# Token mix of a fused attention and channel-mix kernel: U times the tokens in plain fp32 on 32-column tiles, summed by VectorE, and one product with V's high and low half on the partitions

## What is computed

```python
def _moe2_ref(x, U, V, w_ch1, w_ch2):          # x is (4, 576, 512), U (576, 32), V (32, 576)
    xt = x.transpose(0, 2, 1)
    h = xt @ U @ V                             # per batch: tokens reduced to 32 rows, and spread again
    u = x + h.transpose(0, 2, 1)
    ch = np.maximum(u @ w_ch1, 0.0) @ w_ch2
    return (u + ch).astype(np.float32)
```

## Time and profile before

| | |
|---|---|
| median of 3 runs | 800.24 us (797.22 to 801.04) |
| profiled execution | 798.4 us, its span 796.6 us |
| granted TensorE clock, mean | 0.994 of full speed |
| busy, TensorE / weight loads | 759.2 us (95%) / 666.6 us (84%) |
| busy, VectorE / ScalarE / GpSimd | 335.2 / 299.9 / 153.1 us |
| chain that ended last, TensorE's share | 87% |

### The profile page before, as it was taken

One profiled execution on the slowest core, in us unless ns is written; L12 is line 12 of the kernel. 1 busy time (PEld: TensorE's weight loads), 2 busy tenths in 40 slices (PEclk: granted clock), 3 DMA queues, 4 the chain that ended last, 5 costly groups with the idle time before them and its releaser, 6 DMA issues.

```text
span 796.6 us, 13313 instructions
## 1 busy us (share of the span) xinstructions
PE 759.2 (95%) x5040; PEld 666.6 (84%) x5040; DVE 335.2 (42%) x706; ACT 299.9 (38%) x787; POOL 153.1 (19%) x168
## 2 busy tenths in 40 slices
PE   4689899999999999899999999999999999999998
PEld 2567788888888888778899999899899889899997
DVE  6758776767576836765411211121131122113111
ACT  4647676666777655533433110110110111111110
POOL 5777220302011214300565100000000000000000
PEclk9979999999999999999999999999999999999999
DMA  7863342323233101000243100010010001001001
GB/s 141 198 159 61 66 78 47 62 53 70 43 60 62 51 1 53 1 27 1 82 132 105 38 2 1 1 39 0 0 39 0 0 0 39 0 0 41 1 0 40
DMA packets 121748, 35.77 MB, mean 45 GB/s; under 512 B 109536, under 2 KB 115680, under 8 KB 121696
## 3 DMA queue, kind: packets, MB, share of 16 engines
q1 hardware_dynamic: 112000, 34.02, 17.6%
q10 hardware_dynamic: 9696, 1.05, 0.9%
HBM read 30.33 MB, written 4.72 MB: 44 GB/s over the span
## 4 chain that ended last, share of the span: by engine, by line
PE 87%; DVE 6%; issue 2%; ACT 2%; SPq 1%; DMA 0%; ACTq 0%; DVEq 0%
PE bank L1193 27%; PE bank L1195 26%; PE bank L1194 26%; PE bank L1245 2%; PE bank L1234 2%; PE bank L1214 2%; SPq L471 1%; DVE sq L1051 1%; PE bank L1274 1%; DVE sq_l L1055 1%; DVE xf L1041 1%; PE bank L1333 1%; DVE probs L994 1%; PE bank L1347 1%; PE bank L1334 1%
## 5 line engine op out<-in xcount | busy, mean ns | idle before, releaser
L1163 DVE SCALAR_TENSOR_TENSOR h_l<-bank,h_h 128x384 fp32r<-128x384 f32 x96 | 53.5, 558 | 308.9 <-ACT h_h L933 308.9
L933 ACT ACTIVATE h_h<-bank 128x384 fp32r<-128x384 f32 x96 | 47.2, 492 | 333.5 <-PE bank L1195 333.4
L1193 PE MATMUL bank<-ut_h,w_h 128*128 128x384 f32 x384 | 130.5, 340 | 0.0
L1195 PE MATMUL bank<-ut_h,w_l 128*128 128x384 f32 x384 | 129.4, 337 | 0.0
L1194 PE MATMUL bank<-ut_l,w_h 128*128 128x384 f32 x384 | 129.0, 336 | 0.0
L1195 PE MATMUL bank<-w_h,h_l 128*128 128x512 f32 x288 | 113.8, 395 | 0.0
L1194 PE MATMUL bank<-w_l,h_h 128*128 128x512 f32 x288 | 113.6, 395 | 0.0
L1193 PE MATMUL bank<-w_h,h_h 128*128 128x512 f32 x288 | 112.0, 389 | 0.0
L1193 PE MATMUL bank<-xs_h,wk_h 128*128 128x256 f32 x288 | 86.3, 300 | 1.8 <-DVE xs_l L1121 1.8
L1194 PE MATMUL bank<-xs_l,wk_h 128*128 128x256 f32 x288 | 81.8, 284 | 0.0
L1195 PE MATMUL bank<-xs_h,wk_l 128*128 128x256 f32 x288 | 81.6, 283 | 0.0
(11 more groups left out here) (124 smaller groups left out, 1253.0 us busy)
## 6 DMA issues: line engine op xcount, KB each, us to landing
stage<-in_moe_w_ch_dram SPq DMA_DIRECT2D x16, 512.0 KB, 3.4
out_dram<-result SPq DMA_DIRECT2D x18, 256.0 KB, 2.1
q_raw<-in_q_dram SPq DMA_DIRECT2D x64, 40.0 KB, 2.1
q_raw<-in_q_dram SPq DMA_DIRECT2D x64, 32.0 KB, 2.1
v_raw<-in_v_dram SPq DMA_DIRECT2D x32, 64.0 KB, 2.4
k_raw<-in_k_dram SPq DMA_DIRECT2D x48, 40.0 KB, 2.1
k_raw<-in_k_dram SPq DMA_DIRECT2D x52, 32.0 KB, 2.1
stage<-in_moe_w_k_dram SPq DMA_DIRECT2D x3, 512.0 KB, 3.9
```

What stands on the lines that cost most here:

```text
L933: act.activation(h_h[:, m % KRING, :], h_bank[m % 2][:, 0:C2], ACT.Relu).then_inc(hh_done, 1)
L1163: dve.scalar_tensor_tensor(h_l[:, m % KRING, :], h_bank[m % 2][:, 0:C2], 0.0, h_h[:, m % KRING, :].bitcast(F32), op0=ALU.max, op1=ALU.subt ...
L1193: pe.matmul(dst, lhs[0], rhs[0], start=start, stop=False)
L1195: return pe.matmul(dst, lhs[1], rhs[0], start=False, stop=stop)
```

## The change

The reduction takes x as it lies, in plain fp32, and U in plain fp32 with 32 columns (u_pad). Product i of the 20 pairs goes to the 32 columns (and the 32 rows of g_bank) number i mod 4, so a batch's five products lie on four parts; each part is a partial sum. ScalarE moves part 0 into SBUF (move), VectorE adds the parts 1, 2 and 3 to it one after another (sum). ScalarE writes the high part of the sum twice, rows 0 to 31 and 64 to 95 (high), VectorE the low part, rows 32 to 63 and 96 to 127 (low). V stands once: its high part on rows 0 to 63, its low part on rows 64 to 127 (vp), so one product per pair takes the place of two. The splits of x and of U are gone. U is loaded by its own routine into a buffer that GpSimd clears ahead of its first weight split, at the same place of SP's queue, and doesn't take a weight buffer; V's piece and all later ones are numbered one lower and so swap buffers. The slots of all steps are new. In the channel mix all engines take the steps LATE + m behind step m, m = 0 to 5; before, they were at several places around steps 0 and 1.

Left out here: declarations, the loops that call `mix_steps` with a slot in place of a list, and the constants of the pieces.

```diff
@@ -174,10 +174,17 @@
-X_SLOT = [1, 2, 3, 3, 4, 4, 5, 7, 8, 10, 11, 12, 13, 13, 14, 16, LATE, LATE]
-G_SLOT = [n + 1 for n in X_SLOT]
-H_SLOT = [7, 8, 10, 11, 11, 12, 12, 13, 16, 16, 17, 17, 18] + [LATE + 3] * (NTILE - 13)
-X2RING = 3
+PARTS = [(b, n, b * S // P + n) for b in range(B) for n in range(S_TILES)]
+G_SLOT = [1] * (2 * S_TILES) + [5] * S_TILES + [13, 13, 13, LATE, LATE]
+MOVE_SLOT = [2, 2, 6, LATE]
+SUM_SLOT = [2, 3, 6, LATE]
+HIGH_SLOT = [3, 4, 7, LATE + 1]
+LOW_SLOT = [3, 4, 7, LATE + 1]
+H_SLOT = [5, 6, 7, 8, 9, 10, 11, 12, 13, 14, 15, 16, 17, LATE + 3, LATE + 3, LATE + 4, LATE + 4, LATE + 5]
+U_SLOT = [n + 1 if n < LATE else n for n in H_SLOT]
+LATE_STEPS = max(U_SLOT) - LATE + 1
...
@@ -187,22 +194,12 @@
-LAST_TILE = {(b * S + S - 1) // P: b for b in range(B)}
-def mix_steps(engine, slots):
-    steps = []
-    for n in slots:
-        if engine == "vector":
-            steps += [("u", t) for t in range(NTILE) if H_SLOT[t] + 1 == n]
-        if engine in ("scalar", "vector"):
-            steps += [("gs", b) for t, b in LAST_TILE.items() if G_SLOT[t] + 1 == n]
-            steps += [("x", t) for t in range(NTILE) if X_SLOT[t] == n]
-        if engine == "tensor":
-            steps += [("g", t) for t in range(NTILE) if G_SLOT[t] == n]
-            steps += [("h", t) for t in range(NTILE) if H_SLOT[t] == n]
-    return steps
+def mix_steps(engine, slot):
+    tables = {"tensor": [("g", G_SLOT), ("h", H_SLOT)],
+              "scalar": [("move", MOVE_SLOT), ("high", HIGH_SLOT)],
+              "vector": [("u", U_SLOT), ("sum", SUM_SLOT), ("low", LOW_SLOT)]}
+    return [(kind, i) for kind, table in tables[engine] for i, n in enumerate(table) if n == slot]
...
@@ -518,17 +513,17 @@
+    def load_u():
+        sp.wait_ge(u_zero, 1)
+        u_even, u_odd = u_pad[:, 0, :, :], u_pad[:, 1, :, :]
+        sp.dma_start(u_even[:, 0:S_FULL, :], u_in[0:FULL, :].rearrange("(t p) r -> p t r", p=P)).then_inc(u_landed, 16)
+        sp.dma_start(u_even[0:TAIL, S_FULL, :], u_in[FULL:S, :]).then_inc(u_landed, 16)
+        sp.dma_start(u_odd[TAIL:P, 0, :], u_in[0:TAIL, :]).then_inc(u_landed, 16)
+        sp.dma_start(u_odd[:, 1:S_TILES, :], u_in[TAIL:S, :].rearrange("(t p) r -> p t r", p=P)).then_inc(u_landed, 16)
...
@@ -648,6 +643,7 @@
+    pool.memset(u_pad[:, :, :, :].rearrange("p a t r -> p (a t r)"), 0.0).then_inc(u_zero, 1)
...
@@ -668,29 +664,17 @@
-    pool.wait_ge(w_split, NB_PIECES)
-    pool.memset(stage[PIECE_U % 2][:, 0:2 * S_TILES * RANK], 0.0).then_inc(u_zero, 1)
-    for c in range(1, 4):
+    for c in range(1, NC1 - 1):
-    pool.wait_ge(stage_in[PIECE_U % 2], STAGE_COUNT[PIECE_U])
-    raw = stage[PIECE_U % 2][:, 0:2 * S_TILES * RANK].rearrange("p (t r) -> p t r", r=RANK)
-    us = u_split[:, :, :, :].rearrange("p a t r -> p (a t) r")
-    step(pool.tensor_copy(us[:, :, 0:RANK], raw))
-    pool.tensor_copy(us[:, :, 2 * RANK:3 * RANK], raw)
-    pool.tensor_tensor(us[:, :, RANK:2 * RANK], raw, us[:, :, 0:RANK].bitcast(F32), ALU.subtract)
-    pool.tensor_tensor(us[:, :, 3 * RANK:4 * RANK], raw, us[:, :, 0:RANK].bitcast(F32), ALU.subtract)\
-        .then_inc(w_split, 1)
-    for c in range(4, NC1 - 1):
-        make_xr(c)
-    step(pool.memset(vp_h[:, :].bitcast(F32), 0.0))
-    step(pool.memset(vp_l[:, :].bitcast(F32), 0.0))
+    step(pool.memset(vp[:, :].bitcast(F32), 0.0))
-    step(pool.tensor_copy(vp_h[:, DH:DH + S], raw))
-    pool.tensor_tensor(vp_l[:, DH:DH + S], raw, vp_h[:, DH:DH + S].bitcast(F32), ALU.subtract)\
+    step(pool.tensor_copy(vp[:, DH:DH + S], raw))
+    pool.tensor_tensor(vp[DH:P, DH:DH + S], raw[DH:P], vp[DH:P, DH:DH + S].bitcast(F32), ALU.subtract)\
+    pool.wait_ge(w_split, PIECE_V + 1)
...
@@ -804,19 +788,18 @@
-    def mix_step(kind, t):
-        if kind == "x":
-            wait(act, x2_done, t + 1)
-            if t == 0:
+    def mix_step(kind, b):
+        if kind == "move":
+            if b == 0:
-            if t >= X2RING:
-                act.wait_ge(g_mm, t - X2RING + 1)
-            act.activation(x2_h[:, t % X2RING, :].rearrange("p (a b) -> p a b", a=KT), xcols(t * P, P), ACT.Copy)\
-                .then_inc(x2h_done, 1)
+            if b >= 2:
+                act.wait_ge(gl_done, b - 1)
+            act.wait_ge(g_mm, S_TILES * (b + 1))
+            act.activation(g_sums[RANK:2 * RANK, b % 2, :], g_bank[b % 2][0:RANK, :], ACT.Copy).then_inc(g_moved, 1)
-            b = t
-            act.wait_ge(g_mm, batch_tiles(b)[-1][0] + 1)
-            act.activation(g_split[:, b, :], g_bank[b % 2][:, :], ACT.Copy).then_inc(gh_done, 1)
+            act.wait_ge(g_summed, 3 * b + 3)
+            act.activation(g_split[0:RANK, b, :], g_sums[0:RANK, b % 2, :], ACT.Copy)
+            act.activation(g_split[2 * RANK:3 * RANK, b, :], g_sums[0:RANK, b % 2, :], ACT.Copy).then_inc(gh_done, 1)
...
@@ -933,8 +912,8 @@
-            if weights and m == 0:
-                for step in mix_steps("scalar", [LATE + 2]):
+            if weights and m < LATE_STEPS:
+                for step in mix_steps("scalar", LATE + m):
...
@@ -1065,17 +1044,20 @@
-        if kind == "gs":
-            dve.wait_ge(gh_done, t + 1)
-            dve.tensor_tensor(g_split[DH:P, t, :], g_bank[t % 2][DH:P, :],
-                              g_split[DH:P, t, :].bitcast(F32), ALU.subtract).then_inc(gl_done, 1)
-            return
-        dve.wait_ge(x2h_done, t + 1)
-        if t >= 2:
-            dve.wait_ge(g_mm, t - 1)
-        dve.tensor_tensor(x2_l[:, t % 2, :].rearrange("p (a b) -> p a b", a=KT), xcols(t * P, P),
-                          x2_h[:, t % X2RING, :].bitcast(F32).rearrange("p (a b) -> p a b", a=KT),
-                          ALU.subtract).then_inc(x2l_done, 1)
+        part = [slice(RANK * n, RANK * n + RANK) for n in range(4)]
+        b, sums = t, g_sums[:, t % 2, :]
+        if kind == "sum":
+            dve.wait_ge(g_moved, b + 1)
+            dve.tensor_tensor(sums[part[2], :], sums[part[1], :], g_bank[b % 2][part[1], :], ALU.add).then_inc(g_summed, 1)
+            dve.wait_ge(g_summed, 3 * b + 1)
+            dve.tensor_tensor(sums[part[3], :], sums[part[2], :], g_bank[b % 2][part[2], :], ALU.add).then_inc(g_summed, 1)
+            dve.wait_ge(g_summed, 3 * b + 2)
+            dve.tensor_tensor(sums[part[0], :], sums[part[3], :], g_bank[b % 2][part[3], :], ALU.add).then_inc(g_summed, 1)
+        else:
+            dve.wait_ge(gh_done, b + 1)
+            for rows in (part[1], part[3]):
+                ins = dve.tensor_tensor(g_split[rows, b, :], sums[part[0], :], g_split[part[0], b, :].bitcast(F32), ALU.subtract)
+            ins.then_inc(gl_done, 1)
...
@@ -1156,15 +1138,12 @@
-            if token_mix and m < 2:
-                for step in mix_steps("vector", [LATE + 4 * m]):
-                    mix_step(*step)
-            if token_mix and m == 0:
-                for step in mix_steps("vector", [LATE + 2]):
+            if token_mix and m < LATE_STEPS:
+                for step in mix_steps("vector", LATE + m):
...
@@ -1321,19 +1300,19 @@
-    def reduce_tokens(t):
-        if t == 0:
-            pe.wait_ge(w_split, PIECE_U + 1)
-        pe.wait_ge(x2l_done, t + 1)
-        for b, slot, _ in where[t]:
-            if slot == 0 and b >= 2:
-                pe.wait_ge(gl_done, b - 1)
-            lhs = u_split[:, b % 2, slot, :]
-            pe.matmul(g_bank[b % 2][:, :], lhs, x2_h[:, t % X2RING, :], start=slot == 0, stop=False)
-            ins = pe.matmul(g_bank[b % 2][:, :], lhs, x2_l[:, t % 2, :], start=False,
-                            stop=slot == S_TILES - 1)
-        ins.then_inc(g_mm, 1)
+    def reduce_tokens(i):
+        b, slot, t = PARTS[i]
+        if i == 0:
+            pe.wait_ge(u_landed, 4 * 16)
+        if slot == 0 and b >= 2:
+            pe.wait_ge(g_summed, 3 * (b - 1))
+        wait(pe, x2_done, t + 1)
+        rows = slice(RANK * (i % 4), RANK * (i % 4) + RANK)
+        pe.matmul(g_bank[b % 2][rows, :].rearrange("p (a b) -> p a b", a=KT), u_pad[:, b % 2, slot, :], xcols(t * P, P),
+                  start=slot < 4, stop=slot + 4 >= S_TILES).then_inc(g_mm, 1)
...
@@ -1344,9 +1323,7 @@
-            pe.matmul(mix_bank[t % 2][:, :], vp_h[:, col:col + P], g_split[:, b, :], start=n == 0, stop=False)
-            ins = pe.matmul(mix_bank[t % 2][:, :], vp_l[:, col:col + P], g_split[:, b, :], start=False,
-                            stop=n == len(parts) - 1)
+            ins = pe.matmul(mix_bank[t % 2][:, :], vp[:, col:col + P], g_split[:, b, :], start=n == 0, stop=n == len(parts) - 1)
...
@@ -1388,8 +1365,8 @@
-            if weights and m < 2:
-                for step in mix_steps("tensor", [LATE + 1 + 2 * m]):
+            if weights and m < LATE_STEPS:
+                for step in mix_steps("tensor", LATE + m):
```

More of the change, by code:

```diff
@@ L165 @@
 SPLIT1 = {piece: n + 1 for n, piece in enumerate(PIECES1)}
-PIECE_U, PIECE_V = NB_PIECES, NB_PIECES + 1
-FIRST2 = NB_PIECES + 2
+PIECE_V = NB_PIECES
+FIRST2 = NB_PIECES + 1
 N_PIECES = FIRST2 + M2
@@ L224, in build @@
```

(35 more changed lines are left out.)

## The result

The changed kernel took **788.18 us** (median of 5 runs, 787.44 to 791.88), the kernel before beside it 798.73 (5 runs): ratio 0.9872, interval 0.9842 to 0.9903. The forecast was 788.0 us. The profiled execution took 787.75 us, its span 785.7, at a mean granted clock of 0.996; the sum had given it 786.2. So the total is within 2 us, and the question is whether its terms were. Against each other the medians differ by 10.6 us, where the forecast had 12.2: it was put on the 800.24 us of the first 3 runs of the kernel before, and with 2 more runs that median is 798.73.

The account below looks back on a forecast made before the run. TensorE's queue between 300 and 400 us was taken as the bound. -4.65 - 1.7 - 2.3 - 4.4 - 0.6 + 1.5 = -12.2 us, put on the 800.24 us median, gave 788.0 us; range 784.5 to 797.

Parts of the forecast that it names:

- The spread: Token mix, products with V: 40 become 20 at 0.233 us each, gaining 4.65 us of TensorE work.
- The reduction: Products with U: 9.3 us becomes 7.0, four column tiles at a time plus 1.0 for switches; gain 2.3 us.
- No overlap: Rival, 0.12: four streams over the same rows aren't served at once; reduction 18.4 us, total 799.4 us, no change.
- Strict order: Rival, 0.13: passes start in queue order, so second passes hold next products; reduction 11.3 us, total 792.3 us.
- Drained passes: Rival, 0.08: each product's increment makes the next wait for its end; 0.63 us a pass, total 807 us.
- The waits for tokens, 4.4 us, and for mix_bank, 1.7: TensorE's waits in the token mix for VectorE's token low halves and additions of V products go, restarts included.
- New waits, 1.5 us: Token mix: VectorE's new sums and halves, queued before squares TensorE wants, cost 1.5 us; bounds 0 and 5.
- the square's, half of 1.15 left: TensorE's wait for a square's low half, 1.15 us: half counted as gone, gain 0.6 us; bounds 0 and 1.15.
- It is a tie: Behind unit 6: VectorE finishes the squares by 4.8 us, TensorE wants that square at 4.7.
- VectorE late: Rival, 0.07: overlap as forecast, but each chain stands before squares TensorE wants; 5 us instead of 1.5, total 791.5 us.
- The piece FIRST2+4: Channel mix: this weight piece's split is done some 1 us before its unit; under 1 us if wrong.
- at a time when nobody waits: U's split leaves GpSimd, listed among the items at no cost; no change expected before 300 us.

Follow-up runs that it names:

- e_spread_twice: Changed kernel with each of the 20 products with V done twice into the same bank: 793.13 us, ratio 0.9942.
- e_one_tile: Changed kernel with all 20 products with U on column tile 0, VectorE's additions all reading that part: 801.91 us, ratio 1.0055.
- e_sum2_later: Changed kernel with batch 2's move, sums, high and low halves in slots 11 and 12 instead of 6 and 7: 785.25 us, ratio 0.9844.
- e_split_later: Changed kernel with ScalarE's high half of weight piece FIRST2+1 behind unit 3 of chunk 8, so GpSimd's low half comes later: 787.69 us, ratio 0.9882.
- e_usplit_back: Changed kernel with GpSimd's four operations of U's split put back where they stood, result unused: 790.83 us, ratio 0.9912.
- e_tile_by_tile: Changed kernel with the products with U ordered by column tile inside a slot instead of by turns: 791.87 us, ratio 0.9941.
- e_spread_alone: Kernel before the change with the product with vp_l left out, in the old slots: 796.94 us, ratio 0.9979.

## Why the prediction was right in its total, step by step

- **The bound** (TensorE's queue between 300 and 400 us): right. VectorE's 0.7 and ScalarE's 4.3 us less of busy time show nowhere.
- **The spread, 4.65 us of work:** right. From start to next start, the 40 products with V took 10.2 us without their waits, the 20 of now take 5.0. e_spread_twice puts the 4.65 back and finds them, less what fills pauses.
- **The reduction, 7.0 us:** right, 6.9 (7.3 with the late product behind each run), and for the reason given: four at a time. *No overlap* would have been 18.4 us with the changes of form; e_one_tile has 17.6 from first start to next start and 18.0 with the late entries, and ends where that rival said no gain would be left. *Strict order* would have taken 11.3; the four records that start at once exclude it. The Trainium skill, TensorE: Matmul & The Clock Gate, section The mechanism, holds that matmuls start strictly in program order; between column tiles the trace differs, and the measurement decides. The estimate of 1.8 us more from the Trainium skill, TensorE: Matmul & The Clock Gate, section Measured speedup vs the span model (3.07 for 4), wasn't borne out: a round of four takes 0.86 us, as one product does alone. *Drained passes* fell with the same rows.
- **The waits for tokens, 4.4 us, and for mix_bank, 1.7:** they went, but for one wait of 1.1 us at 331.25, of another cause than theirs.
- **New waits, 1.5 us, and the square's, half of 1.15 left: this step failed.** By starts, TensorE's pauses in this stretch cost 7.3 us before and 1.3 + 2.8 + 1.0 = 5.1 after. The sum had 0.6 + 1.5 = 2.1, so it was 3 us too kind, inside its own bounds of 0 and 5 and at their upper end. The place was named ("It is a tie", slots 8 and 9 with GpSimd's operations), but the price was put at a part of two chains. What the count of the tie left out is how far the delay carries: VectorE waits 2.18 us for the move and then has no idle time in which to catch up, so the sums and low halves hold up the squares of units 7 and 8 as well, and the second of these then meets GpSimd's 2.4-us operations (e_sum2_later takes both waits away, e_split_later the share of one GpSimd operation, 2.1 us). That is the rival *VectorE late* in mechanism; by size VectorE's two pauses are 4.1 us, where that rival with the square's 0.6 had 5.6. I had named 3 us for sq_l as its sign; 2.5 were seen.
- **The piece FIRST2+4:** no wait. The one of 0.7 us stands at GpSimd's half of FIRST2+2 at 377.45, a step earlier: the mechanism right, the piece wrong, 1.0 us with the restart.
- **"A change before 300 us, where I expect none"; "at a time when nobody waits":** wrong, by 1.1 us to the good. TensorE waited there for VectorE, which GpSimd's split of U held up, as e_usplit_back shows.
- **The sum with measured terms:** -4.65 - 2.0 (reduction, 9.3 for 7.3) - 1.9 (pauses, 7.3 for 5.1 and 0.3 in short delays that show no idle time, at 326.88 and 366.91) = -8.55; the token mix shows -8.5. With -1.1 from U's split and -1.3 of scatter at the start it makes the 10.9. So the hit in the total has two unforeseen gains, one of them chance, that stand against 3 us of waits too few, and a third piece of luck: 788.0 stood on the median of 3 runs of the kernel before, 1.5 us above that of 5, and so took up most of the 1.6 us by which the difference of the medians fell short.

## What to carry to other kernels

When a change takes work out of the bound engine's queue, the engines that feed it keep their times, so count what they deliver and when, instant by instant, before the full work is written down as gain; and where your count says "a tie", price it as a loss. A moved operation of GpSimd's is priced by what VectorE does at that instant, not by who waits for its output. For a product with few columns of weights, plain fp32 on four column tiles taken by turns costs two passes for four products.

## What the runs showed of the hardware

- **GpSimd stretches some of VectorE's operations and not others.** An operation with two operands in SBUF went from 0.42 to 2.20 and 2.52 us (128x256), a pair of 32x512 from 1.38 to 4.65, a tensor-scalar operation on 128x4 elements from 0.16 to 0.85; the reciprocal of 128x4, at 158.37 us with GpSimd's last operation of U's split beside it, stayed at 0.18. The addition from PSUM (L1040) took 0.68 in both surroundings.
- **Column tiles overtake the queue, within a limit.** By turns 10 products take 2.70 us, tile by tile 3.63, on one tile 8.70.
- **A pause can be followed by half the clock.** In e_usplit_back, e_tile_by_tile and e_one_tile the pause of some 2.9 us for sq_l was followed by a stretch at half of the clock; in the changed kernel, with the same pause, it was not. In e_spread_alone waits of 1.2 and 0.6 us, at 344.09 and 345.61, came before such a stretch. The stretches of e_usplit_back (granted clock in the third column from the right):

```profile
333.00:337.00 4.00, 2.91 (x19) 2.44 (x18) 3.93 (x6) 3.72 (x6) 2.83 (x2) 1.00 0.00 0
337.00:341.00 4.00, 1.47 (x7) 0.90 (x6) 3.94 (x4) 0.34 (x1) 2.55 (x2) 1.00 0.02 7
341.00:345.00 4.00, 4.00 (x14) 3.22 (x13) 1.98 (x3) 0.00 (x0) 0.00 (x0) 0.57 0.38 124
345.00:349.00 4.00, 4.00 (x35) 3.91 (x34) 3.64 (x8) 1.61 (x4) 0.00 (x0) 1.00 0.00 0
```

TensorE was busy 1.47 of 4 us; then the granted clock is 0.57, that is 1.2 GHz for most of the next 4 us, while products of 128x512 start 0.43 apart, not 0.233, and then 2.4 GHz again. It costs 1.5 us beyond the pause: the token mix is 171.0 us in e_usplit_back and 169.5 in the changed kernel, with the same waits. Why the pause brings it in one execution and not in another stays open.
